# Attention and experts on one core: the first q and k chunk turned tile by tile, and eight scatters of one lot with no weight splits between them

## What is computed

```python
scores = scale * q @ k.T, masked to 0 <= i - j < 64      # 8 heads of 64
attn_out = softmax(scores) @ v                            # 2304 x 512
noisy = x @ w_gate + log1p(exp(x @ w_noise)) * noise      # 8 experts
top2 = two largest of noisy, softmax over the two
out[tok] += top2_w * (relu(x[tok] @ w1[e]) @ w2[e])       # 512 -> 1024 -> 512
h = out @ w_in; g = h * clip(h + 3, 0, 6) / 6; y = g @ w_out   # 512 -> 2048 -> 512
```

## Time and profile before

| what | value |
|---|---|
| median of 3 runs (lowest, highest) | 1018.68 us (1015.92, 1020.06) |
| the profiled execution: its time, its span | 1019.22 us, 1017.5 us |
| PE busy in the span | 988.1 us, 97% |
| PE busy, 0 to 140 us of the span | 116.3 us of 140 |
| POOL busy, 90 to 150 us | 53.3 us of 60 |
| mean granted TensorE clock | 0.991 of full speed |

### The profile page before, as it was taken

One profiled execution on the slowest core, in us unless ns is written; L12 is line 12 of the kernel. 1 busy time (PEld: TensorE's weight loads), 2 busy tenths in 40 slices (PEclk: granted clock), 3 DMA queues, 4 the chain that ended last, 5 costly groups with the idle time before them and its releaser, 6 DMA issues.

```text
span 1017.5 us, 18019 instructions
## 1 busy us (share of the span) xinstructions
PE 988.1 (97%) x7108; PEld 877.5 (86%) x7108; DVE 417.8 (41%) x897; ACT 227.7 (22%) x537; POOL 423.5 (42%) x326
## 2 busy tenths in 40 slices
PE   7989889999999999999999999999999999999998
PEld 6777668989889898989989989999999999999997
DVE  3578764313222222213222255545445445355333
ACT  4666521111111111111111121111111211111111
POOL 3067976993855739192855729101101001000000
PEclk9999879999999999999999999999999999999999
DMA  9699876764452716263342433200101111000000
GB/s 181 128 207 247 271 258 222 246 186 150 135 185 90 230 61 208 70 180 122 125 145 86 151 106 125 64 32 21 42 31 41 41 31 41 31 1 1 32 1 31
DMA packets 125878, 115.94 MB, mean 114 GB/s; under 512 B 64912, under 2 KB 93520, under 8 KB 125808
## 3 DMA queue, kind: packets, MB, share of 16 engines
q1 hardware_dynamic: 106368, 75.36, 27.0%
q10 hardware_dynamic: 13680, 20.75, 6.0%
q0 software_dynamic: 5760, 18.88, 5.8%
HBM read 75.90 MB, written 39.06 MB: 113 GB/s over the span
## 4 chain that ended last, share of the span: by engine, by line
PE 81%; SPq 7%; POOL 5%; DMA 3%; issue 2%; DVE 1%; ACT 0%; ACTq 0%; POOLq 0%; DVEq 0%
PE PS L1635 20%; PE PS L1755 20%; PE PS L1739 19%; PE PS L1618 19%; SPq L500 3%; SPq L490 3%; POOL x_sorted L711 3%; PE PS L1602 1%; POOL W L690 1%; POOL W L680 1%; PE PS L1680 1%; DMA x_sorted<-zeros 1%; DMA y_sorted<-y_sb 0%; PE PS L1498 0%; DMA stage<-in_moe_w_dram 0%
## 5 line engine op out<-in xcount | busy, mean ns | idle before, releaser
L1635 PE MATMUL PS<-W,hs_room 128*128 128x512 f32 (+1 forms) x960 | 245.2, 399 | 0.1
L1618 PEld LDWEIGHTS PS<-xs,W 128*128 128x128 f32 x1536 | 231.0, 189 | 10.8 <-issue 0.2
L1618 PE MATMUL PS<-xs,W 128*128 128x256 f32 (+2 forms) x1536 | 239.7, 307 | 0.0
L1755 PE MATMUL PS<-W,gs 128*128 128x512 f32 x864 | 217.0, 396 | 0.9 <-DVE gs L1353 0.9
L1739 PE MATMUL PS<-x2s,W 128*128 128x384 f32 x1152 | 216.6, 337 | 0.0
L1739 PEld LDWEIGHTS PS<-x2s,W 128*128 128x128 f32 x1152 | 201.4, 188 | 7.2
L680 POOL TENSOR_TENSOR W<-stage,ones_f 128x1024 fp32r<-128x1024 f32 (+1 forms) x100 | 147.6, 1484 | 136.5 <-PE PS L1635 133.1
L1635 PEld LDWEIGHTS PS<-W,hs_room 128*128 128x128 f32 (+1 forms) x960 | 172.3, 186 | 34.6 <-DVE hs_room L1203 0.3
L1755 PEld LDWEIGHTS PS<-W,gs 128*128 128x128 f32 x864 | 161.5, 188 | 31.5 <-issue 1.6
L690 POOL TENSOR_TENSOR W<-stage,W 128x1024 fp32r<-128x1024 f32 (+1 forms) x100 | 185.4, 1863 | 5.8
L1203 DVE SCALAR_TENSOR_TENSOR hs_room<-PS,hs_room 128x256 fp32r<-128x256 f32 (+2 forms) x128 | 61.9, 484 | 290.6 <-ACT hs_room L899 290.6
(11 more groups left out here) (133 smaller groups left out, 574.4 us busy)
## 6 DMA issues: line engine op xcount, KB each, us to landing
stage<-in_moe_w_dram SPq DMA_DIRECT2D x64, 512.0 KB, 4.2
x_sorted<-zeros SPq DMA_DIRECT2D x7, 1280.0 KB, 7.6
y_sorted<-y_sb ACTq DMA_DIRECT2D x33, 256.0 KB, 3.7
x_in<-x_sorted ACTq DMA_DIRECT2D x31, 256.0 KB, 4.3
vD<-in_v_dram SPq DMA_DIRECT2D x72, 64.0 KB, 2.8
out_dram<-o_sb SPq DMA_DIRECT2D x18, 256.0 KB, 2.1
stage<-in_moe_w_in_dram SPq DMA_DIRECT2D x8, 512.0 KB, 3.9
stage<-in_moe_w_out_dram SPq DMA_DIRECT2D x8, 512.0 KB, 3.8
```

Source lines behind the costliest of these rows:

```text
L1618: last = nc.tensor.matmul(HP_[:, c % 2, 0:n], W[:, par, 0, b, at:at + P], xs[part][:, a, kd, 0:n], start=start, stop=(kd == KD - 1 and (a, ...
L1635: last = nc.tensor.matmul(Y[0:n, first + t, :], hs[:, c % 2, a, t * P:t * P + n], W[:, par, 1, b, c * DM:(c + 1) * DM], start=(c == 0 and ...
L1755: last = nc.tensor.matmul(OP[:, tt, :], gs[:, c % 2, a, tt * P:(tt + 1) * P], W[:, 1, c // FC, b, at:at + DM], start=(c == 0 and (a, b) == ...
```

## The change

It has five parts. (1) Chunk 0 of q and k is waited for and turned by tiles (`turn_tile(r)`, all heads) in place of halves of the heads; scores(0) stands between the two; item 2 is turned into the banks of `OUT`, so that it waits for no exponentials; transpose_p(0, 0) and move_pt(0, 0) stand earlier, and DVE's row_max(0) before its second move. v tile 0 is issued on ACT's queue, v tile 1 on SP's before chunk 3. (2) Chunks 4 and 8 lie within one batch and are loaded with two transfers each for q and k in place of three; SP raises the semaphore by the missing 32. (3) The gates' weights are loaded on POOL's queue. (4) Chunks 3 and 4 of the weights are split behind lot 2 (`SPLIT_AT`), and chunk 7 is issued in iteration 17. (5) Tile 5's and 6's scatters come one iteration earlier, with pauses in place of splits, and lot 2's eight stand one behind the other, with two keep_x among them.

```diff
--- before.py
+++ after.py
@@ -85,8 +85,8 @@
     RAWS = 4
-    FIRST_AT = (4, 6, 8, 10, 12, 13, 14, 15)
-    SPLIT_AT = (7, 8, 11, 12, 13)
+    FIRST_AT = (4, 6, 8, 10, 12, 13, 14, 17)
+    SPLIT_AT = (7, 8, 11)
     PIECES = 4
@@ -95,7 +95,8 @@
     ZERO_AT = (16, 17)
     ZERO_PARTS = 4
-    SCATTER_AT = {8: 0, 9: 1, 10: 2, 12: 3, 13: 4, 14: 5, 15: 6}
+    SCATTER_AT = {8: (0,), 9: (1,), 10: (2,), 12: (3,), 13: (4, 5), 14: (6,)}
     CHUNKS = N // CT
     ITEMS = 2 * CHUNKS
     AHEAD = 3
...
...
@@ -398,17 +403,19 @@
         def raw_count(c):
-            return sum(32 * len(list(pieces(n))) for n in range(1, c + 1) if raw_slot(n) == raw_slot(c))
+            return sum(32 * (3 - n % 2) for n in range(1, c + 1) if raw_slot(n) == raw_slot(c))
         def item_buf(n):
-            return n % 2 if n < 2 else max(n - AHEAD, 0) % 2
+            return n % 2 if n < 2 else (n - AHEAD) % 2
+        def item_bank(n, side):
+            return PS[:, 5 + side, :] if n == 2 else SC[:, item_buf(n), side, :]
         def items_before(T):
-            return 2 if T < 2 else min(T + AHEAD - 1, ITEMS)
+            return T + 1 if T < 2 else min(T + AHEAD - 1, ITEMS)
         def item_at(T):
             return T + AHEAD if T + AHEAD < ITEMS else None
@@ -416,13 +423,15 @@
         def turned(n, side, h, r):
-            return SC[:, item_buf(n), side, :].rearrange("p (h s r w) -> p h r s w", h=2, s=2, r=TK)[:, h, r]
+            return item_bank(n, side).rearrange("p (h s r w) -> p h r s w", h=2, s=2, r=TK)[:, h, r]
         def moved_from(n, side):
-            return SC[:, item_buf(n), side, :].rearrange("p (h s m) -> p h s m", h=2, s=2)
+            return item_bank(n, side).rearrange("p (h s m) -> p h s m", h=HP if n < 2 else 2, s=2)
         def ring(n, side):
+            if n < 2:
+                return qkT[:, :, side, :, n, :]
             c, hh = divmod(n, 2)
             first = 2 * c % RB
             return qkT[:, 2 * hh:2 * hh + 2, side, :, first:first + 2, :].rearrange("p h s r w -> p h s (r w)")
@@ -470,6 +479,13 @@
         def unit(e, part, c):
             return 2 * FC * e + FC * part + c
+        def load_v_block(eng, t, s):
+            b, i = half(t, s)
+            for x in range(2):
+                eng.dma_start(vD[WIN * x:WIN * (x + 1), t % RV, s, :, 0:D],
+                              v[b].rearrange("(h x) r d -> x r h d", x=2)[x, i * WIN:(i + 1) * WIN])\
+                    .then_inc(v_full[t % RV], 16)
         w1_c = w1.rearrange("e (c p) f -> (e c) p f", p=P)
         w2_c = w2.rearrange("e (c n p) d -> (e c) p n d", n=2, p=P)
@@ -490,16 +506,15 @@
                         sp.dma_start(raw_place(c, side)[p0:p0 + np_, r].rearrange("p (h d) -> p h d", d=D),
                                      src[b, :, row:row + np_, :].rearrange("h p d -> p h d"))\
                             .then_inc(raw_full[raw_slot(c)], 16)
+                if c % 2 == 0 and not crossed(c):
+                    sp.sem_inc(raw_full[raw_slot(c)], 32)
             def load_v(t):
                 if t >= RV:
                     sp.wait_ge(out_full, t - RV + 2)
                 for s in range(2):
-                    b, i = half(t, s)
-                    for x in range(2):
-                        sp.dma_start(vD[WIN * x:WIN * (x + 1), t % RV, s, :, 0:D],
-                                     v[b].rearrange("(h x) r d -> x r h d", x=2)[x, i * WIN:(i + 1) * WIN])\
-                            .then_inc(v_full[t % RV], 16)
+                    load_v_block(sp, t, s)
             def load_first(c):
                 if c >= QCH:
@@ -518,18 +533,15 @@
                 sp.wait_ge(sc_full, T + 1)
             both = ((0, q), (1, k))
-            for hh in range(2):
-                for r in range(TK):
+            for r in range(TK):
+                for hh in range(2):
                     sp.dma_start(q_raw[:, 0, r, DM // 2 * hh:DM // 2 * (hh + 1)].rearrange("p (h d) -> p h d", d=D),
                                  q[0, HP * hh:HP * (hh + 1), r * P:(r + 1) * P, :].rearrange("h p d -> p h d"))\
-                        .then_inc(raw_first[hh], 16)
+                        .then_inc(raw_first[r], 16)
             load_qk(1, both)
             load_qk(2, both)
-            load_v(0)
+            load_v(1)
             load_qk(3, both)
-            load_v(1)
-            for n, w in enumerate((wg, wn)):
-                sp.dma_start(wgn[:, :, n * E:(n + 1) * E], w.rearrange("(k p) e -> p k e", p=P)).then_inc(s_small, 16)
             load_v(2)
...
@@ -712,6 +724,9 @@
                                         out_offset=bass.IndirectOffsetOnAxis(ap=slot_cur[:, k, t:t + 1], axis=0),
                                         in_=x_cur[:, t, :], in_offset=None).then_inc(x_sent[n], 16)
+            for n, w in enumerate((wg, wn)):
+                nc.gpsimd.dma_start(wgn[:, :, n * E:(n + 1) * E], w.rearrange("(k p) e -> p k e", p=P)).then_inc(s_gates, 16)
             pool.wait_ge(m_all, 5)
             def keep_x(t):
                 pool.wait_ge(out_moved, t + 1)
@@ -733,34 +748,33 @@
             for T in range(2, max(SCATTER_AT) + 1):
                 keep_x(T - 2)
-                if T in SCATTER_AT:
-                    scatter(SCATTER_AT[T], 0)
+                transfers = [(t, k) for t in SCATTER_AT.get(T, ()) for k in range(2)]
+                if transfers:
+                    scatter(*transfers[0])
                 if T in SPLIT_AT:
                     first_there(SPLIT_AT.index(T))
                     split_hi(0, SPLIT_AT.index(T), PIECES)
-                elif T in SCATTER_AT:
-                    pause()
-                if T in SCATTER_AT:
-                    scatter(SCATTER_AT[T], 1)
+                for t, k in transfers[1:]:
+                    if T not in SPLIT_AT:
+                        pause()
+                    scatter(t, k)
                 if T in SPLIT_AT:
                     split_lo(0, SPLIT_AT.index(T), SPLIT_AT.index(T) + 1, PIECES)
-            c = len(SPLIT_AT)
-            first_there(c)
-            for n in range(2 * PIECES):
-                if n < PIECES:
-                    split_hi(0, c, PIECES, n, n + 1)
-                else:
-                    split_lo(0, c, c + 1, PIECES, n - PIECES, n - PIECES + 1)
+            kept = max(SCATTER_AT) - 1
+            for n in range(2 * LOTS[FIRST_LOT][1]):
                 scatter(LOTS[FIRST_LOT][0] + n // 2, n % 2)
-            for c in range(len(SPLIT_AT) + 1, SCH):
+                if n % 4 == 3:
+                    keep_x(kept)
+                    kept += 1
+            for c in range(len(SPLIT_AT), SCH):
                 first_there(c)
                 split_hi(0, c, PIECES)
                 split_lo(0, c, c + 1, PIECES)
-                if c == len(SPLIT_AT) + 1:
-                    for t in range(max(SCATTER_AT) - 1, TILES - 1):
-                        keep_x(t)
-            keep_x(TILES - 1)
+                if kept < TILES:
+                    keep_x(kept)
+                    kept += 1
+            assert kept == TILES
             for t in range(LOTS[FIRST_LOT + 1][0], TILES):
                 for k in range(2):
                     scatter(t, k)
@@ -854,9 +868,13 @@
                 nc.scalar.activation(dst, src, func).then_inc(act_done, 1)
             nc.scalar.preload_act_table_set("natural_log_exp_and_others")
+            load_v_block(act, 0, 0)
             move_first(0)
+            load_v_block(act, 0, 1)
             move_first(1)
             exps(0)
+            move_pt(0, 0)
             move_first(2)
             def load_x(e, j):
                 row, n = e * ROOM + block_row(e, j), block_rows(e, j)
@@ -874,7 +892,7 @@
                     move_first(item_at(T))
                 for n in due(T, 3):
                     route(n, 0)
-                if T < TILES:
+                if 1 <= T < TILES:
                     move_pt(T, 0)
                 if T >= 2:
                     move_xt(T - 2)
...
@@ -1161,8 +1179,8 @@
                     step(nc.vector.tensor_tensor(gate[:, 1, tiles], gap[:, 1, m], gap[:, 2, m], ALU.mult))
             move_second(0)
+            row_max(0)
             move_second(1)
-            row_max(0)
             row_max(1)
             move_second(2)
             dve.wait_ge(s_const, 4)
@@ -1405,21 +1423,25 @@
             def turn_qk(n, i=None):
                 c, hh = divmod(n, 2)
-                if c == 0:
-                    pe.wait_ge(raw_first[hh], 64)
-                elif hh == 0:
+                if hh == 0:
                     pe.wait_ge(raw_full[raw_slot(c)], up(raw_count(c), i, 8 * (3 - c % 2)))
-                if n >= 2:
-                    pe.wait_ge(sc_act, up(max(n - AHEAD, 0) + 1, i))
-                if n == AHEAD:
-                    pe.wait_ge(ld_act, AHEAD)
-                    pe.wait_ge(ld_dve, AHEAD)
+                if n >= AHEAD:
+                    pe.wait_ge(sc_act, up(n - AHEAD + 1, i))
                 carried(i)
                 for side in range(2):
```

(13 more changed lines are left out.)

14 lines of the change are left out of this document (7 added, 7 removed).

## The result

The changed kernel takes 1022.54 us, median of 8 runs (1021.18 to 1025.14), beside 1018.90 (8 runs, 1015.92 to 1021.23) for the kernel before: a ratio of 1.0040, 95% interval 1.0023 to 1.0057. The prediction said 1015.9 us, range 1012.6 to 1020.2. The time lies outside it and the sign is wrong: the kernel is some 3.6 us slower. The profiled executions stand 3.1 us apart (1022.32 us, span 1020.5, before 1019.22 and 1017.5), so the two traces show most of the difference. I read them in the order in which the work runs.

What follows compares the result with a forecast made beforehand. PE, idling only in the first 140 us, and the chain through POOL's last scatter were both taken as critical. L - D + clock = 3.1 - 6.9 + 1.0 = -2.8 gave 1015.9 us, range 1012.6 to 1020.2.

Steps and rivals of the forecast that it cites:

- L: Time by which POOL takes longer from lot 2's places to its last scatter: 3.1 us, with cases of 1 and 5.
- D: Time by which lot 2's places come earlier: 6.0 + 0.9 = 6.9 us, between 3.3 and 8.5.
- clock: Lower PE clock after the wait near 170 us in expert 0: 1.0 us, as half a chance of the middle.
- the step on SP's queue: SP 6.0 us earlier at chunk 5, with 2.7 from chunk 4's fewer transfers; lower end 3.3 if paced by bytes.
- the start's 2.6: First exponentials 1.0 us earlier, and the time between them and the second 1.6 us shorter.
- rival 4: Start's waits only move to chunk 1's and 2's landing while SP's part works: D = 4, 1018.8 us; chance 0.15.
- the prediction's own lower case: At the start, v tile 0 on ACT's queue delays chunk 1, leaving a gain of 1.0 us.
- two sums agreed on 6.0: SP's queue gave 6.0 us; PE's start and two waits for k, 2.6 + 1.64 + 1.99, gave 6.2; 6.0 was taken.
- DVE beside splits: DVE routes lot 2 faster with chunks 3 and 4's splits moved away: 0.9 us, range 0 to 2.
- Rival 2: Five splits beside lot 4's routing lengthen DVE's small instructions, 5 to 6 us in all: 1017.5 us; chance 0.10.
- up to 4.8: PE's wait before expert 0's blocks 3 and 4 and at the next gate: up to 1.7 + 3.1 = 4.8 us.
- (3): POOL's list gates and byte-bound transfers keep the attention's gain from arriving, D under 3.1: 1021.8 or 1025.2 us; chance 0.15.

Runs made afterwards that it cites:

- v_on_sp: Changed kernel with v's tile 0 loaded from SP's queue behind chunk 2, not from ACT's at the start; ratio 1.0056 to the kernel before.
- attention_v: Changed kernel's attention side with POOL's list of before, and v's tile 0 on SP's queue behind chunk 2; ratio 0.9994 to the kernel before.
- spaced: Changed kernel with one 0.6 us POOL copy between lot 2's scatters; ratio 1.0067 to the kernel before, repeated 1.0065.
- split_at_14_shift: Changed kernel with a fourth split in iteration 14 and 32 DVE semaphore increments in the preamble; ratio 1.0002 to the kernel before.
- code_shift: Changed kernel with 32 DVE semaphore increments, which nothing waits for, in its preamble; ratio 1.0038 to the kernel before.
- pool_only: Kernel before with only the change's POOL list (two splits moved behind lot 2, eight scatters in a row); ratio 1.0082 to the kernel before.
- filled: Changed kernel with 48 extra matmul calls of zeros before PE turns expert 0's blocks 3 and 4; ratio 1.0169 to the kernel before.
- split_at_14: Changed kernel with chunk 3 split in iteration 14; ratio 1.0000 to the kernel before.
- after_again: Changed kernel run once more, unchanged, on another chip; ratio 1.0048 to the kernel before.
- filled_again: Second run of filled, the changed kernel with 48 extra matmul calls of zeros; ratio 1.0158 to the kernel before.
- zeros_and_14: Changed kernel with a fourth split in iteration 14 and the last two y_sorted zeroings ahead of the second expert's chunks; ratio 1.0014 to the kernel before.
- zeros_early: Changed kernel with the last two y_sorted zeroings issued ahead of the second expert's weights; runs 1027.67 to 1056.95 us; repeated, ratio 1.0140 to the kernel before.
- zeros_spread: Changed kernel with y_sorted's four zeroings issued in attention iterations 5, 7, 9 and 11; ratio 1.0137 to the kernel before.
- groups 1, 2 and 4: Follow-up kernels, each group on one chip beside its own runs of the kernel before: 1024.71, 1023.74 and 1022.32 us.
- groups 3 and 5: Follow-up kernels, each group on one chip beside its own runs of the kernel before: 1019.60 and 1019.10 us.
- attention_only: Changed kernel's attention side with POOL's list of before; ratio 0.9952 to the kernel before, repeated 0.9984.
- code_shift_again: Second run of code_shift, the changed kernel with 32 DVE semaphore increments in its preamble; ratio 1.0052 to the kernel before.

## Why the prediction was wrong

The forecast sum was L - D + clock = 3.1 - 6.9 + 1.0 = -2.8. The trace has 3.3 - 4.5 + 1.0, which is -0.2, and 3.0 for what the sum lacked: 2.7 for the last scatter's landing and 0.3 for the padding behind it. That makes +2.8, and the project stands 2.84 us later. In the prediction's words, the 15.1 us from POOL's last scatter to the project, which it moved along unchanged, became 19.2 (166.09 to 185.28).

1. **D, the step on SP's queue, failed: 4.5 where 6.9 stood.** I let chunk 4 "take what chunk 3 took", 2.7 us less for two transfers less. It took 0.7 less. The rows of before allowed either reading and I had the right one as the lower end, 3.3 for SP; SP's gain at chunk 5 was 3.15. The other half of the step, the start's 2.6 as PE's side of D, was put together wrongly, 2.0 + 0.0 in the trace and not 1.0 + 1.6, and went at chunk 2's landing, as rival 4 had it. What kept most of the 1.6 away was chunk 1's k behind v's bytes, the prediction's own lower case: in v_on_sp the time between the two exponentials is 2.9 us and not 4.12. v_on_sp and attention_v show that bringing this landing forward by 1.4 us only passes the wait on. That two sums agreed on 6.0 was no support: both rested on k arriving.

2. **DVE beside splits, mis-sized the other way: 1.9, not 0.9.** The lot's routing lost 1.9 us less beside an idle POOL (of D's 4.5, 2.6 stand at the scores: 98.79, before 101.36). Rival 2's mechanism is true as well: beside the splits `hot` of lot 4 took 0.84 for two (140.26) against 0.42 in the earlier trace rows. It cost nothing in this trace, since lot 4's places stood at 145.53 and POOL came to lot 4 only at 156.21. The rule of the Trainium skill's "SBUF — State Buffer" that I had weighed agrees with the trace in both places: `gap` of lot 2 took 0.17 us with no split beside it, 1.42 before.

3. **L was right**, 3.3 for 3.1, and the list of 56.7 us to 0.2 us. spaced shows the list on the path; split_at_14_shift shows that most of its price returns when it is shortened.

4. **What failed most is a term that wasn't there: from the last scatter's end to its landing.** I moved the 1.7 us of before (2.70 less the scatter's 0.97) along with the scatter. It became 4.4, 2.7 more. The padding behind it landed 7.3 us after its issue at 172.25, 6.98 before. Two conditions go with the late landing. In every trace with the fourteen in a row *and* y_sorted's zeroings beside them POOL waits 4.66 to 5.95 us (the changed kernel, code_shift twice, pool_only, v_on_sp, filled, split_at_14_shift, spaced twice). Where idle time of 3 us or more stands ahead of lot 4, zeroings or not, it is 2.08 to 2.19 (before, the three kernels with the attention part alone, split_at_14, after_again, filled_again, zeros_and_14, zeros_early twice). With fourteen in a row and no zeroing, 2.45 (zeros_spread). The last rests on one trace of a kernel whose time was off. The prediction had counted each scatter's 1.26 us on POOL, and never the 262144 bytes that it hands on: in 1.28 us that is 205 GB/s, and the engines moved 333 to 342 in all. Nor had it followed `w_ready` through SP's queue, which carried the zeroings along with the splits. It named SP's queue only for the attention. What the landing costs in the end is read from traces; no run took it away alone. And it is the make-up of this one execution: in after_again the landing was prompt, DVE's stop made the routing late in its place, and the ratio was 1.0048.

5. **The waits inside expert 0**: 12.24 us and not "up to 4.8". The 4.8 was 1.7 + L, and left out the late landing and that PE had more to give back. It came to blocks 3 and 4 at 161.09 and not at 173.13, 12.0 us earlier, where D + 1.7 is 8.6 as forecast and 6.2 with the D of the trace. Beside the wait for rows, the kernel before had lost 2.61 us to DVE's logits ahead of 132.22, and its first product had run at the lower clock, 3.90 us and not 2.25.

6. **The clock** cost about what was taken, 1.0, and this is partly luck. From block 4's turns to the project PE took 10.6 us, before 8.9: its 9 products took 3.69 us in place of 2.33, at a granted clock of 0.57. That is 1.65 more, nearly the 1.7 of which the forecast took a chance. But the padding landed at 179.6, and before, the project stood 4.7 us behind that landing. By this estimate it could not have stood before 184.2, so only some 1.0 of the 1.65 reached it. That any of it would have been saved by filling the wait was not shown.

Of the rivals, (3) is nearest in time (1021.8) but wrong in mechanism: D was not under L, the last scatter was earlier. It was (4) for D with a landing that no rival had.

Better than both kernels is the attention part with the old list: 0.9952, 0.9984, and, with v on SP, 0.9994. The first two intervals lie under 1, the third doesn't. The sign is settled for the attention part without v's move, its size is not.

## What to carry to other kernels

When a list of transfers is packed closer together, add up the bytes per time beside it and the time of the last landing, not only the issuing engine's time; the slack between two bursts (8.38 us here) stood between landings of 6.0 to 6.9 us and of 2.7 to 4.0. When work moves that another queue's waits are tied to (`w_ready`), follow that queue to everything behind the wait. And fewer transfers of the same bytes may win little: here 0.7 of 2.7 us, with the DMA engines at a share of 0.96 from 31 to 37 us.

## What the runs showed of the hardware

**A stop of VectorE that I can't explain.** DVE's timeline of after_again:

```profile
117.02 0.15 DVE L1179 TENSOR_TENSOR gate<-gap 128x4 f32<-128x4 f32 x1
124.33 0.69 DVE L1086 TENSOR_REDUCE negmax<-PS 128x4 f32<-128x512 f32 x1 [7.16 <-remote]
```

row_max(17) waits for the scores, which PE had ended by 117.3; nothing in the profile stands between. The stop is in all eleven traces of groups 1, 2 and 4 with the dense eight scatters (5.60 to 8.68 us), always at this instruction, and in none of groups 3 and 5, nor in the first trace. attention_only, in group 1, has none. So it comes with certain chips and, as far as this one comparison within a chip tells, with the new list of GpSimd. My theory of instructions fetched late fell: code_shift_again, with DVE's code 32 places on, has it at the same row_max(17), in DVE's timeline:

```profile
122.35 0.69 DVE L1089 TENSOR_REDUCE negmax<-PS 128x4 f32<-128x512 f32 x1 [7.20 <-remote]
```

Nor do the zeroings make it (zeros_spread has 7.81). Whether the scatters' spacing does stays open: spaced ran twice on chips without it.

**Two make-ups, one ratio.** Without the stop, and with the list as changed, PE waits 10.94 and 12.24 us ahead of blocks 3 and 4; with it 0.29 us (after_again) and none for x_in (code_shift_again), since PE itself comes late. Yet the changed kernel loses about the same, 1.0040 and 1.0038 without it, 1.0048 and 1.0052 with it.
